# Two more tile buffers in an expert's weight space, in a kernel of decay attention, experts and a SOLU layer

## The reference

```python
# attention with decay: B=2, H=8, S=768, D=48
for t in range(S):
    cur = einsum('bhd,bhe->bhde', u * k[t], v[t])
    y[t] = einsum('bhd,bhde->bhe', r[t], state + cur)
    state = w * state + einsum('bhd,bhe->bhde', k[t], v[t])
x = y.transpose(0, 2, 1, 3).reshape(1536, 384)
# mixture of experts: E=8, D=384, F=1024, capacity 384, one expert a token
expert = argmax(x @ w_gate); gate = its softmax probability
disp[e, slot] = x[i]                      # first come, first served, up to the capacity
out[i] = gate[i] * (relu(disp[e] @ w1[e]) @ w2[e])[slot]
# dense layer
h = out @ w_in;  solu = h * softmax(h);  ln = (solu - mean) / sqrt(var + 1e-6) * g_ln
result = ln @ w_out
```

## Time and profile before

| | us |
|---|---|
| median of 3 runs | 335.09 (333.76 to 336.6) |
| the profiled execution | 335.23 |
| its span, first to last instruction | 333.5 |
| PE busy | 310.2 (93%) |
| DVE busy | 212.7 (64%) |
| ACT busy | 196.4 (59%) |
| POOL busy | 187.0 (56%) |
| first matmul of the experts (L1372) | at 85.02 |

### The profile page before, as it was taken

One profiled execution on the slowest core, in us unless ns is written; L12 is line 12 of the kernel. 1 busy time (PEld: TensorE's weight loads), 2 busy tenths in 40 slices (PEclk: granted clock), 3 DMA queues, 4 the chain that ended last, 5 costly groups with the idle time before them and its releaser, 6 DMA issues.

```text
span 333.5 us, 7114 instructions
## 1 busy us (share of the span) xinstructions
PE 310.2 (93%) x2660; PEld 279.4 (84%) x2662; DVE 212.7 (64%) x471; ACT 196.4 (59%) x374; POOL 187.0 (56%) x168
## 2 busy tenths in 40 slices
PE   7697978988999999999999999799999999999991
PEld 4486767867999999999999999688999999999991
DVE  7764763789855656464554556889897666656610
ACT  2485774878585766766676757256556445533520
POOL 4865677872698988989898969400031111111131
PEclk9999997999999999999999999989999999999998
DMA  8999999994397939494766685000000000000010
GB/s 136 155 261 245 251 226 182 279 398 154 115 372 264 337 130 342 127 300 176 242 197 225 212 266 187 1 0 1 2 25 26 24 24 26 24 26 24 25 44 33
DMA packets 62901, 50.70 MB, mean 152 GB/s; under 512 B 42512, under 2 KB 58256, under 8 KB 62864
## 3 DMA queue, kind: packets, MB, share of 16 engines
q1 hardware_dynamic: 59104, 45.25, 47.2%
q0 software_dynamic: 1920, 4.73, 3.9%
q10 hardware_dynamic: 1840, 0.21, 0.8%
HBM read 38.37 MB, written 11.82 MB: 150 GB/s over the span
## 4 chain that ended last, share of the span: by engine, by line
PE 78%; issue 8%; POOL 7%; DVE 3%; ACT 1%; DMA 1%; POOLq 0%; SPq 0%; DVEq 0%
PE ps L1372 25%; PE ps L1648 15%; PE ps L1665 15%; PE ps L1373 12%; PE ps L1674 3%; POOL own_place L568 2%; PE ps L1445 2%; POOL own_place L575 2%; POOL place L583 1%; PE ps L1366 1%; PE ps L1494 1%; PE ps L1505 1%; POOL place L611 1%; DMA wsq<-in_w_dram 1%; PE ps L1570 1%
## 5 line engine op out<-in xcount | busy, mean ns | idle before, releaser
L511 POOL TENSOR_TENSOR w_lo<-w_raw,w_hi 128x768 fp32r<-128x768 f32 x33 | 60.5, 1859 | 10.3 <-DVE w_lo L517 9.8
L1372 PE MATMUL ps<-xe,w_hi 128*128 128x448 f32 x192 | 61.9, 378 | 0.3
L1372 PE MATMUL ps<-h,w_hi 128*128 128x448 f32 x192 | 61.8, 378 | 0.0
L1665 PE MATMUL ps<-w_hi,h 128*128 128x384 f32 x192 | 51.5, 340 | 0.0
L1373 PE MATMUL ps<-h,w_lo 128*128 128x224 f32 x192 | 50.7, 264 | 0.0
L1373 PE MATMUL ps<-xe,w_lo 128*128 128x224 f32 x192 | 50.7, 264 | 0.0
L1648 PE MATMUL ps<-w_hi,xe 128*128 128x512 f32 x144 | 47.7, 402 | 2.0 <-DVE xe L1219 2.0
L672 POOL TENSOR_TENSOR rstd<-var_b,minus_half 128x1 f32<-128x1 f32 x12 | 6.8, 565 | 74.6 <-DVE var_b L1318 74.6
L954 DVE TENSOR_TENSOR ps<-ps,rk_in 128x448 f32<-128x448 f32 x32 | 20.2, 632 | 32.9 <-ACT rk_in L726 32.9
L1372 PEld LDWEIGHTS ps<-xe,w_hi 128*128 128x128 f32 x192 | 36.0, 188 | 5.0 <-issue 2.0
L517 POOL TENSOR_TENSOR w_lo<-w_raw,w_hi 128x1024 fp32r<-128x1024 f32 x16 | 38.2, 2411 | 1.9 <-DVE w_lo L517 1.9
(11 more groups left out here) (165 smaller groups left out, 612.3 us busy)
## 6 DMA issues: line engine op xcount, KB each, us to landing
w_raw<-in_moe_w_dram SPq DMA_DIRECT2D x15, 1536.0 KB, 7.8
x_slots<-zeros SPq DMA_DIRECT2D x6, 768.0 KB, 6.0
rk_in<-in_r_dram SPq DMA_DIRECT2D x12, 192.0 KB, 5.3
rk_in<-in_k_dram SPq DMA_DIRECT2D x12, 192.0 KB, 5.9
v_in<-in_v_dram SPq DMA_DIRECT2D x12, 192.0 KB, 5.2
out_dram<-zeros SPq DMA_DIRECT2D x1, 2304.0 KB, 8.1
w_raw<-in_moe_w_dram SPq DMA_DIRECT2D x3, 512.0 KB, 5.3
rows_in<-x_slots SPq DMA_DIRECT2D x8, 192.0 KB, 8.0
```

What stands on the lines that cost most here:

```text
L511: eng.tensor_tensor(w1_lo[:, :, cols], w1_raw[:, i, :, cols], w1_hi[:, :, cols].bitcast(F32), ALU.subtract).then_inc(g.w1_lo, 1)
L1372: pe.matmul(ps[:, bank, 0:2 * n], w_hi, x[:, c, 0:2 * n], start=first, stop=False, skip_group_check=True)
L1665: last = pe.matmul(ps[:, OB + i, 0:DM], ht[:, f, i * P:(i + 1) * P], wt[:, f, :], start=(f == 0 and z == 0), stop=(f == KF - 1 and z == 2))
```

## The change

The kernel gets NB = 6 sets of buffers for the tiles. Four stay where they are; sets 4 and 5 lie in w1_raw[:, 1], the place of the second expert's w1 (more_in, with rk_of and v_of to find a set). So the load of that w1 moves: from behind w2 of expert 0 to behind the loads of expert 0's rows, with a wait for the last tile (y_done, NT). The pads of the two new sets are cleared by DVE in one memset after put_first_diagonal, and TensorE waits for it once, at tile 4.

SP now loads six tiles before the first two parts of zeros; then, as before, a tile and a part take turns, so that the last part of zeros stands behind tile 9 instead of tile 7. A load waits for the tile six before it.

POOL does at most one scatter in an iteration and none in the last one. DVE does decay_r ahead of add_own in each tile from the second on.

```diff
-    NB = 4
+    NB = 6
+    IN_PLACE = 4
...
-        rk_in = sb("rk_in", [P, NB, 2, H, DP])
-        v_in = sb("v_in", [P, NB, H, DP])
+        rk_in = sb("rk_in", [P, IN_PLACE, 2, H, DP])
+        v_in = sb("v_in", [P, IN_PLACE, H, DP])
...
+        more_in = w1_raw[:, 1].rearrange("p c f -> p (c f)")[:, 0:(NB - IN_PLACE) * 3 * H * DP]\
+            .rearrange("p (a b h d) -> p a b h d", a=NB - IN_PLACE, b=3, h=H)
+
+        def rk_of(i):
+            return rk_in[:, i] if i < IN_PLACE else more_in[:, i - IN_PLACE, 0:2]
+
+        def v_of(i):
+            return v_in[:, i] if i < IN_PLACE else more_in[:, i - IN_PLACE, 2]
...
             for a in range(1, ZERO_PARTS):
                 zero_slots(a)
-                load_tile(NB - 1 + a)
-            for t in range(NB - 1 + ZERO_PARTS, NT):
+                load_tile(NB + a - 1)
+            for t in range(NB + ZERO_PARTS - 1, NT):
                 load_tile(t)
             for a in range(KD):
                 load_first_w1(a)
             load_w2(0, 0)
-            load_w1(1, 1)
...
             sp.wait_ge(scattered, 16 * LATE[0])
             load_rows(0, 0)
+            sp.wait_ge(y_done, NT)
+            load_w1(1, 1)
...
-                for _ in range(2):
-                    if t >= GROUPS[group_of(stored)][-1] + 4:
-                        if stored == 0:
-                            pool.wait_ge(slots_zeroed, 16 * ZERO_PARTS)
-                        scatter(stored)
-                        stored += 1
+                if t < NT - 1 and t >= GROUPS[group_of(stored)][-1] + 4:
+                    if stored == 0:
+                        pool.wait_ge(slots_zeroed, 16 * ZERO_PARTS)
+                    scatter(stored)
+                    stored += 1
...
+            dve.memset(more_in.rearrange("p a b h d -> p (a b h) d")[:, :, D:DP], 0.0).then_inc(more_pads_ready, 1)
...
                 if 0 < t < NT - 1:
+                    decay_r(t + 1)
                     add_own(t + 1)
-                    decay_r(t + 1)
...
+                if t == IN_PLACE:
+                    pe.wait_ge(more_pads_ready, 1)
```

More of the change, by code:

```diff
@@ L301, in decay_attention_moe_solu @@
         first_odd_ready = sem("first_odd_ready")
+        more_pads_ready = sem("more_pads_ready")
         first_ruk_ready = sem("first_ruk_ready")
@@ L413, in load_tile @@
                 for j, src in ((0, r_v), (1, k_v)):
-                    sp.dma_start(rk_in[:, i, j, :, 0:D], src[b, c]).then_inc(loaded[i], 16)
+                    sp.dma_start(rk_of(i)[:, j, :, 0:D], src[b, c]).then_inc(loaded[i], 16)
                     if t == 0 and j == 0:
@@ L417, in load_tile @@
                         load_w(sp, 1)
-                sp.dma_start(v_in[:, i, :, 0:D], v_v[b, c]).then_inc(v_loaded[i], 16)
+                sp.dma_start(v_of(i)[:, :, 0:D], v_v[b, c]).then_inc(v_loaded[i], 16)
             def load_w1(e, i):
@@ L567, in own_parts @@
                     pool.wait_ge(own_step, 2 * t - 1)
-                pool.tensor_tensor(ru[:], rk_in[:, i, 0, :, 0:D], u_all[:], ALU.mult).then_inc(own_step, 1)
+                pool.tensor_tensor(ru[:], rk_of(i)[:, 0, :, 0:D], u_all[:], ALU.mult).then_inc(own_step, 1)
                 if t == 0:
@@ L574, in own_parts @@
                 pool.wait_ge(own_ready, t)
-                pool.tensor_tensor(ruk[:], ru[:], rk_in[:, i, 1, :, 0:D], ALU.mult).then_inc(own_step, 1)
+                pool.tensor_tensor(ruk[:], ru[:], rk_of(i)[:, 1, :, 0:D], ALU.mult).then_inc(own_step, 1)
             def last_keys(t):
@@ L582, in last_keys @@
                     pool.wait_ge(update_done, updates(t - 2))
-                pool.tensor_tensor(k_last[:, t % 2, :, 0:D], rk_in[:, i, 1, :, 0:D], wlast[:], ALU.mult)\
+                pool.tensor_tensor(k_last[:, t % 2, :, 0:D], rk_of(i)[:, 1, :, 0:D], wlast[:], ALU.mult)\
                     .then_inc(k_last_ready, 1)
@@ L1451, in turn_rk @@
                 pe.wait_ge(loaded[i], 32 * (t // NB + 1))
+                if t == IN_PLACE:
+                    pe.wait_ge(more_pads_ready, 1)
                 if t > 0:
                     pe.wait_ge(r_decayed, t)
-                turn(RT, rk_in[:, i, 0]).then_inc(r_turned, 1)
+                turn(RT, rk_of(i)[:, 0]).then_inc(r_turned, 1)
                 if t == 0:
-                    turn(KT, rk_in[:, i, 1]).then_inc(k_turned, 1)
+                    turn(KT, rk_of(i)[:, 1]).then_inc(k_turned, 1)
                 else:
@@ L1494, in state_update @@
                     last = pe.matmul(ps[part, UB, DP * (h // 2):DP * (h // 2 + 1)], k_last[:, t % 2, h, :],
-                                     v_in[:, t % NB, h, :], start=True, stop=True)
+                                     v_of(t % NB)[:, h, :], start=True, stop=True)
                 last.then_inc(update_done, 1)
@@ L1513, in own_keys_out @@
                 for h in range(H) if t < NT - 1 else EVEN_PAIRS + ODD_PAIRS:
-                    last = pe.matmul(y_place(h), v_in[:, t % NB, h, :],
+                    last = pe.matmul(y_place(h), v_of(t % NB)[:, h, :],
                                      scores[:, t % 2, h % 2, h // 2, :], start=(c == 0 and h < 4), stop=(h >= H - 4),
```

## The result

| | before | changed |
|---|---|---|
| median | 335.85 us (333.76 to 338.5, 4 runs) | 342.45 us (341.49 to 343.14, 4 runs) |
| profiled execution | 335.23 | 342.02 |
| its span | 333.5 | 340.3 |
| first matmul of the experts | 85.02 | 94.87 |
| first matmul of the dense layer | 214.56 | 222.67 |

The ratio is 1.019, 95% interval 1.011 to 1.0271: slower, by 6.6 us, where 5.0 was forecast. The interval is +3.7 to +9.1 us, so these runs don't tell the two apart. An execution more than 1.5% above the fastest of its kernel counts as slow and is left out of every ratio.

The account below looks back on a forecast made before the run. Attention was taken to be paced by the full load queue and POOL, with the experts following almost without a gap. +5.1 - 0.4 + 0.3 = +5.0 us on 335.2 gave 340.2 us; 8 in 10 range 337.0 to 343.0.

Parts of the forecast that it names:

- The zeros: SP's load queue: sixth part of zeros lands at 53.5 us, first scatter at 53.8, next key product +5.1 us.
- The arrival of POOL: POOL before its first scatter: there as early as 39.7 us, then idle for up to 14 us.
- Deep buffers: POOL's three waits for k loads in attention: 7.1 us in all that deeper buffers could give back.
- Low clock: TensorE after its longer idle at the stall: clock of 0.50 as already before, costed at nothing more.
- DVE's order and w1: Late attention and first expert: decay_r first gains 0.4 us (0 to 0.8); late w1 costs nothing, at worst +0.8.
- The end of attention: Ninth scatter and expert 0's rows: one more scatter after the last state decay, +0.3 us out of 0 to +1.3.
- the first term: Delay at the key product of tile 8: scatter 6.4 us later less 1.3 for one scatter fewer, +5.1 us.
- rival 3: Stall plus worse start: rows 1.3 us late, w1 0.8 late, longer low clock; +7 to +9 us, chance 0.10.
- Rival 1: Load queue not bound by engines: zeros come in time, kernel gets faster, 330 us if landing at 43.5; chance 0.10.
- Rival 2: After the stall POOL's own idle times close up, so it is partly made up: about +2.5 us, 337.7; chance 0.12.

Follow-up runs that it names:

- Run 2: The kernel before with only the parts of zeros moved two tiles later in SP's queue; 343.96 us, ratio 1.0292.
- run 1: The changed kernel with the six parts of zeros back at their old places in SP's queue; 334.76 us, ratio 0.9985 to the kernel before.
- run 4: The changed kernel with zeros at their old places and scatters from iteration 7, up to two each; 334.84 us, ratio 0.9999 to the kernel before.
- run 7: The changed kernel with the first scatter in iteration 9, up to two an iteration; 329.54 us on chip B, ratio 0.9885 to the kernel before.
- run 9: The changed kernel with the first scatter in iteration 9, measured again on chip C; 334.93 us, ratio 1.0018 to the kernel before.
- run 10: The changed kernel with the first scatter in iteration 8, up to two an iteration; 333.76 us on chip C, ratio 0.9976 to the kernel before.
- first pair: The first profiles of the kernel before and the changed kernel, without further edit; 335.23 and 342.02 us.
- second pair: The kernel before and the changed kernel, both unedited, profiled once more on chip B; 331.23 and 337.39 us.
- run 3: The kernel before with only expert 1's w1 loaded late and DVE's decay_r ahead of add_own; 335.43 us, ratio 1.0001.
- run 11: The changed kernel with the old rule of up to two scatters an iteration, the last included; 341.68 us, ratio 1.0211 to the kernel before.
- Run 8: The changed kernel with the zeros behind all twelve tiles and nine scatters behind POOL's loop; 333.72 us, ratio 1.005 to the kernel before.

## Why the prediction held

**The zeros.** "I expect the sixth part of zeros at about that time", taken as 53.5: it landed at 53.45, and the scatter started at 53.79 where 53.8 was forecast. The key product behind it came at +5.06, forecast +5.1. Run 2 shows that this order alone makes the loss, run 1 that without it nothing is lost. The argument that carried it, that a full queue conserves its work, is seen again in runs 1 and 4: waits of 8.4 and 9.7 us under two other names, and the same time. That the landing hit to a twentieth of a microsecond is luck, as the 53.5 was the middle of 53.0 to 54.06. The arrival of POOL was off: "as early as" 39.7 us and up to 14 us idle were forecast, 42.5 and 11.26 measured, as waits for TensorE took 2.1 us of what the loads gave. It cost nothing, because the stall swallows it.

**Deep buffers.** That the 7.1 us were "what deeper buffers could give back" holds for the waits (0.5 left) but not as it was meant: run 1 has the deeper buffers and waits 7.2. The waits went because two tiles passed the zeros in the queue. The Trainium skill (DMA: Bandwidth & Descriptors, Rules for kernel authors) advises to issue early and wait late. In this queue, whose share is 1.11, only the second half could be had: what went early pushed something back, and then the wait for what was pushed back has to go later as well. The change did the first without the second. Runs 7, 9 and 10, which do both, have no loss.

**Low clock.** It was costed at nothing more. In the first pair that holds: TensorE wakes at 56.70 and is at 0.50 up to 60, though the rest before it was 10.83 us and not 2.40. In the second pair it doesn't. The change wakes at 56.83 and is still at 0.50 up to 62 us; the kernel before wakes at 50.69 and is back at 0.90 from 54 to 56:

```profile
60.00:62.00 2.00, 2.00 (x30) 2.00 (x32) 0.72 (x2) 1.87 (x6) 0.42 (x1) 0.50 1.00 365
```

```profile
54.00:56.00 2.00, 2.00 (x44) 1.94 (x42) 1.00 (x6) 1.49 (x6) 0.61 (x1) 0.90 1.10 266
```

In that stretch POOL loses 0.9 us: it waits 1.71 us for the state and 1.04 for slot numbers, where the kernel before waited 1.42 and 0.41. Run 2 has the same two waits, 1.72 and 1.00, again with TensorE at 0.50 up to 63 us. That the clock is their reason fits these runs, but none shows it by itself.

**DVE's order and w1.** -0.4 and 0 (at worst +0.8) were forecast, run 3 measured +0.04 us for both (interval -1.0 to +1.1); so neither sign is shown in the time. In POOL's rows the gain is there: from the first scatter to the last state decay it takes 24.83 us in run 3 and 25.31 in the first profile of the kernel before.

**The end of attention.** +0.3 was taken out of 0 to +1.3. In the first pair the ninth scatter was 5.1 us late and the rows 4.4, close to the forecast. In the second pair it was 6.8 and 6.1: the scatter of the kernel before had started 1 us sooner (46.51 against 47.47) and that of the change at nearly the same time (53.91 against 53.79), and the 0.9 us lost in iteration 8 took back what iterations 9 and 11 had gained. So the step that was sized too small is the first term: it is +5.06 in the first pair and +6.15 in the second, where +5.1 was forecast, as it depends on when the zeros of the old kernel come, and I had one execution. A part of rival 3, the longer low clock, is in the second pair; its other two, rows 1.3 us late in full and a late w1, were not found.

**The rivals.** Rival 1 (zeros in time) asked for a queue that isn't bound by its engines; the landing at 53.45, not 48.4, refutes it. Rival 2 (partly made up) was right on one point in the first pair, the waits behind the stall shrink: L624 no longer waits in iterations 9 and 11, and the +5.06 is +4.2 at the last one (in the second pair +6.15 is still +5.95). But the additional scatter takes 0.9 us of that back.

## What to carry to other kernels

In a queue that is always full, moving a transfer forward is the same edit as moving others back; list what every wait needs landed, count the work ahead of each of these transfers, and find the wait that now comes last. If a load is given way, move the consumer of what gave way by as much (here two tiles passed the zeros, and with the first scatter in iteration 8 instead of 6 the loss is gone). And before more buffers are paid for, see whether the load waited for a free buffer or for the engines: SP's queue had one wait of 3.5 us for a buffer here, so by this row more sets could bring 3.5 us at most (an estimate). And that wait was for the last tile, behind all three waits of POOL for k (SP had issued tile 10 by 53.7 and tile 11 at 57.19), so it could not have shortened any of them.

## What was not expected

At the end of attention DVE, ACT and TensorE stand for 2 to 9 us in some executions, for a releaser that the profile only calls "remote". It is in the profiles of all four kernels on chip A, of all three on chip C, and in the first profile of the change, in none of the four on chip B and not in the first of the kernel before. Kernels with and without the change have it: 2.2 us in run 3, 3.9 in run 1, 8.6 in run 9, most of it at instructions of the last tiles (masks, logits, ranks). POOL goes on, and the DMA engines have room. Every one of these waits is for a semaphore that only TensorE's matmuls raise. In six of the eight profiles TensorE also has idle time put down to "issue" inside a run of matmuls; in runs 3 and 11 its matmuls look whole and only the signal is late (in run 3 the last matmul that raises it ended at 75.29, and DVE went on at 77.76). So what is late is TensorE, and DVE and ACT wait for it. Run 8, on chip B, has such a gap too, 1.49 us at 64.58, though no "remote" wait. Why TensorE is late I can't say; no run removed it.

It comes in attention's fastest versions as well: run 7 and run 9 are one kernel, 2.6 us under the kernel before on one chip and 0.3 over it on another. That the stand took the gain is likely but not shown, as the kernel before was not profiled on chips A and C and may have it there too. It follows the chip or the session rather than the kernel.

In the profile of the kernel before there is another oddity: a DVE instruction on 12 elements a row that took 5.14 us while POOL's subtractions ran. In the changed kernel the same line took 1.50:

```profile
207.31 5.14 DVE L1242 TENSOR_SCALAR ngate<-gate 128x12 f32<-128x12 f32 x1
```

```profile
217.17 1.50 DVE L1255 TENSOR_SCALAR ngate<-gate 128x12 f32<-128x12 f32 x1
```

It made the kernel before lose 2.00 us ahead of the dense layer (its L1648 waited that long for DVE), so that the dense layer starts only 8.11 us later in the changed kernel and not 9.85. Behind that wait the kernel before ran at a lower clock, and the changed one did not, which brings the difference to 6.8 us in the span:

```profile
216.00:220.00 4.00, 4.00 (x12) 3.10 (x12) 2.60 (x6) 3.75 (x8) 0.00 (x0) 0.60 0.00 0
```

```profile
224.00:228.00 4.00, 4.00 (x20) 3.29 (x19) 4.00 (x8) 4.00 (x9) 0.00 (x0) 1.00 0.00 0
```

So two odd stretches nearly cancel. They made the first pair look right in sum and wrong in the middle, and a second pair was needed to see it.
